# Attention values with the exponentials stationary on the whole array, in a fused attention and expert kernel

## The reference

```python
batch, n_heads, seq, head_dim = (4, 8, 768, 64)
ub = np.sum(np.maximum(q[..., None, :] * k_min, q[..., None, :] * k_max), axis=-1)
top_chunks = np.argsort(np.where(causal, ub, -1e9), axis=-1)[..., -6:]
scores = np.where(sel & causal_by_key, (q @ k.T) / 8, -1e9)
attn = np.exp(scores - max); attn /= attn.sum(-1) + 1e-9
x = (attn @ v)                       # 3072 rows of 512
expert = argmax(x @ w_gate); gate = softmax(x @ w_gate)[expert]
# each expert keeps its 80 rows of highest gate:
out[tok] = gate * (relu(x[tok] @ w1[e]) @ w2[e])
```

## Time and profile before

| | |
|---|---|
| median of 3 runs | 266.83 us (266.33 to 269.99) |
| the profiled execution | 266.53 us |
| its span, first to last instruction | 264.8 us |
| granted clock of the span | 1.000 |

### The profile page before, as it was taken

One profiled execution on the slowest core, in us unless ns is written; L12 is line 12 of the kernel. 1 busy time (PEld: TensorE's weight loads), 2 busy tenths in 40 slices (PEclk: granted clock), 3 DMA queues, 4 the chain that ended last, 5 costly groups with the idle time before them and its releaser, 6 DMA issues.

```text
span 264.8 us, 9133 instructions
## 1 busy us (share of the span) xinstructions
PE 256.2 (97%) x3824; PEld 164.4 (62%) x3824; DVE 213.2 (81%) x582; ACT 149.6 (56%) x227; POOL 211.3 (80%) x280
## 2 busy tenths in 40 slices
PE   7799999999999999999999999999999999989993
PEld 7366566666666566666665666656665657676763
DVE  6886696778989988867889889899999998983332
ACT  2295656565667564647584546564856665873320
POOL 6068889998999899897989898979899971726872
PEclk9999999999999999999999999999999999999999
DMA  9989989999799989997999999999799996941782
GB/s 147 189 145 149 235 225 261 228 187 224 125 208 180 209 145 195 173 219 125 215 160 215 171 190 164 215 162 324 142 207 184 328 212 142 165 103 40 136 167 91
DMA packets 148616, 48.34 MB, mean 183 GB/s; under 512 B 131583, under 2 KB 138870, under 8 KB 148512
## 3 DMA queue, kind: packets, MB, share of 16 engines
q1 hardware_dynamic: 135504, 28.73, 54.1%
q0 software_dynamic: 9936, 18.64, 38.6%
q10 hardware_dynamic: 3136, 0.39, 1.0%
HBM read 57.03 MB, written 11.01 MB: 257 GB/s over the span
## 4 chain that ended last, share of the span: by engine, by line
PE 91%; DVE 3%; ACT 2%; DMA 1%; issue 1%; ACTq 1%; POOL 0%; DVEq 0%
PE OB L637 28%; PE SC L546 27%; PE SC L567 7%; PE OB L1395 4%; PE MM L673 4%; PE SC L1369 4%; PE MM L650 3%; PE OB L721 2%; PE MM L474 2%; PE SC L474 2%; PE MM L513 2%; DMA qn<-in_q_dram 1%; ACT EXB L576 1%; PE MM L712 1%; PE MM L982 1%
## 5 line engine op out<-in xcount | busy, mean ns | idle before, releaser
L576 ACT ACTIVATE EXB<-SC 128x1024 f32<-128x1024 f32 (+1 forms) x87 | 83.1, 966 | 35.6 <-PE SC L546 23.9
L602 POOL TENSOR_TENSOR ES<-ES,EXB 128x512 f32<-128x512 f32 (+1 forms) x81 | 84.4, 1044 | 5.1
L546 PE MATMUL SC<-qT,kT 64*128 64x512 f32 (+3 forms) x476 | 86.3, 464 | 0.1
L637 PE MATMUL OB<-EXB,vn 128*64 128x256 f32 (+3 forms) x704 | 72.9, 361 | 0.0
L637 PEld LDWEIGHTS OB<-EXB,vn 128*64 128x64 f32 x704 | 46.1, 137 | 24.0 <-issue 10.4
L546 PEld LDWEIGHTS SC<-qT,kT 64*128 64x128 f32 x476 | 39.2, 187 | 15.8 <-issue 11.5
L602 POOL TENSOR_TENSOR ES<-EXB 128x512 f32<-128x512 f32 (+1 forms) x29 | 45.3, 1561 | 2.4
L586 POOL TENSOR_SCALAR_AFFINE_SELECT EXB<-EXB 128x256 f32<-128x256 f32 x79 | 34.9, 452 | 5.0 <-ACT EXB L576 5.0
L645 ACT ACTIVATE oT<-OB 128x512 f32<-128x512 f32 (+1 forms) x32 | 15.7, 490 | 40.1 <-PE OB L637 40.1
L567 PE MATMUL SC<-unsT,ind 64*128 64x256 bf16 (+5 forms) x238 | 35.6, 295 | 0.1
L567 PEld LDWEIGHTS SC<-unsT,ind 64*128 64x128 bf16 x238 | 11.8, 95 | 15.9 <-issue 7.1
(11 more groups left out here) (270 smaller groups left out, 405.0 us busy)
## 6 DMA issues: line engine op xcount, KB each, us to landing
w1s<-in_moe_w_dram POOLq DMA_DIRECT2D x8, 1024.0 KB, 8.6
w2s<-in_moe_w_dram POOLq DMA_DIRECT2D x7, 1024.0 KB, 13.9
vn<-in_v_dram SPq DMA_DIRECT2D x32, 192.0 KB, 4.5
kn<-in_k_dram SPq DMA_DIRECT2D x62, 96.0 KB, 3.2
qn<-in_q_dram SPq DMA_DIRECT2D x62, 96.0 KB, 3.5
out_dram<-w1s SPq DMA_DIRECT2D x2, 1536.0 KB, 7.2
out_dram<-out_dram SPq DMA_DIRECT2D x2, 1536.0 KB, 9.8
x_rows<-xp SPq DMA_DIRECT2D x7, 384.0 KB, 3.9
```

The source lines that it names most:

```text
L546: op("pe", lambda: pe.matmul(o, kT[j][pr, ts(kt)], qT[j][pr, q0:q1], start=not flags and (not cols or cols[0] == 0), stop=bool(flags)), r= ...
L576: op("act", lambda: ac.activation(Ex(st, None, 0, W), src, ACTF.Exp, scale=SCALE), r=pk, w=[f"E{st}"])
L602: op(e, lambda: sy.queue[e].tensor_tensor(o, in0, in1, ALU.add), r=[f"E{s2}", f"E{first[0]}"] if first else [f"E{s2}"] + kt, w=kt)
L637: op("pe", lambda: pe.matmul(OB[pr, q0:q1], vn[s][:, kt, h, :], ex, start=(n == 0), stop=last), r=[f"vn{s}{h}", "ES0" if st is None else f ...
```

## The change

Values of pairs 0 to 14 are turned round: each 128x128 block of exponentials is stationary on the whole array, and V with a column of ones (128x65) moves. 21 causal blocks of two heads make 42 products for a pair. The output has queries on partitions, and its 65th column is the key sum. DVE divides by it (`rows_out`), transposes the rows in 32x32 blocks into RT for the logit products, and POOL casts them into xp, which now holds four pairs and is written once for a batch. The logit products (`logits`) are eight products on 64x32 tiles with gate weights that are spread out by four more small DMAs at the start; ACT takes them out, POOL adds them up over a batch, and `logits_sum` folds them once for a batch. All folds of exponentials, the key sum products, the row transposes and the copy of OB to oT go, for pairs 0 to 14. The last pair keeps its way. The ranking sort at `i = 12` is issued behind `rows_out`, one 1 MB expert load (`w2_6`) moves from the end of `i = 14` into `i = 15`, the rows of the last batch stay in xp instead of being read back, and gate work that wrote the PSUM tile MM now writes OB. The core of the diff:

```diff
+                vn = [al(pers, "vn", [128, NT, 2, D + 1]) for _ in range(NB)]
...
+                xp = al(pers, "xp", [128, NT, NPB, 128], BF16)
...
+                WB = bass.AP(oT, 0, [[S, 128], [128, NPB], [32, 4], [1, 32]])
+                SEL = bass.AP(oT, 4 * NPB * 32, [[S, 128], [32, 2], [1, 32]])
+                lgp = bass.AP(oT, 4 * NPB * 32 + 64, [[S, 128], [E * 3, NT], [3, E], [1, 3]])
+                LGT = bass.AP(ES, S, [[2 * S, 128], [192, 2], [1, 192]])
+                LGA = bass.AP(w2s[E - 2], 3 * S, [[FB * Dm, 128], [384, 2], [1, 384]]).bitcast(F32)
...
+                for c in range(4):
+                    src = bass.AP(moe_w_gate.tensor, moe_w_gate.offset, [[E, 32], [128 * E, NPB], [32 * E, 4], [1, E]])
+                    dst = WB[c * 32:c * 32 + 32, :, :, c % 2 * E:c % 2 * E + E]
+                    op("sp", lambda: sp.dma_start(dst, src), r=["Wz"], w=[f"Wb{c}"], dsem=f"d_wb{c}")
...
+                    op("dve", lambda: ve.memset(vn[s][:, :, :, D:D + 1], 1.0), w=[f"von{s}"])
...
-                        for h in range(2):
-                            op("pe", lambda: pe.transpose(MB[h * 64:h * 64 + 64, ts(t)], uns[:, t, h, :], ident_bf[:]),
-                               r=["uns", "ident_bf"], w=["MB"], inc=(t == NT - 2 and h == 1))
+                        op("pe", lambda: pe.transpose(MB[:, ts(t)], uns[:, t, :, :].rearrange("p a b -> p (a b)"), ident_bf[:]),
+                           r=["uns", "ident_bf"], w=["MB"], inc=(t == NT - 2))
...
+                def short(i):
                     return 0 < i < NP - 1
-
-                def short(i):
-                    return mid(i) and i != 12 and (i < NPB or i % NPB < 2)
...
-                            if st == 0 and short(i):
-                                rows(i - 1)
...
                         if i == 0 and st == 2:
-                            short_warm()
+                            keep_warm(2, M0, "M0")
...
-                        if i == NP - 2 and st == (4 if short(i) else 5):
-                            wload(E - 2, 1)
-                        if i < NP - 1:
-                            fold(9 - st if st > 3 and short(i) else st, i=i)
-
-                def values(i, bks=(0, 1), ns=(0, 9), out=True):
+                def values(i):
                     s = i % NB
-                    lists = [AVS_LAST[0] if i == NP - 1 else AVS[0], AVS[1]]
-                    order = AV_ORDER if short(i) else [(bk, n) for bk in bks for n in range(len(lists[bk])) if ns[0] <= n < ns[1]]
-                    for g, (bk, n) in enumerate(order):
+                    blocks = [(st, kt, q, c + q * 128 - q0) for st in ((0, 1, 2, 3, 5, 4) if short(i) else range(6))
+                              for kt, q0, q1, c in STEPS[st] for q in range(q0 // 128, q1 // 128)]
+                    for n, (st, kt, q, c) in enumerate(blocks):
+                        first = all(x[2] // 3 != q // 3 for x in blocks[:n])
+                        end = all(x[2] // 3 != q // 3 for x in blocks[n + 1:])
+                        for h in range(2):
+                            o = q // 3 * 512 + (q % 3 * 2 + h) * (D + 1)
+                            op("pe", lambda: pe.matmul(OB[:, o:o + D + 1], Ex(st, h, c, 128), vn[s][:, kt, h, :],
+                                                       start=first and h == 0, stop=end and h == 1),
+                               r=[f"vn{s}{h}", f"von{s}", f"E{st}"], w=[f"O{q // 3}"], inc=end and h == 1)
...
+                def rows_out(i):
+                    b, p = i // NPB, i % NPB
+                    rden, rk = rd(i)
+                    so = bass.AP(OB, D, [[1024, 128], [512, 2], [D + 1, NT]])
+                    xi = bass.AP(OB, 0, [[1024, 128], [512, 2], [D + 1, NT], [1, D]])
+                    rb = bass.AP(rden, 0, [[NT * 2, 128], [NT, 2], [1, NT]])
+                    rx = bass.AP(rden, 0, [[NT * 2, 128], [NT, 2], [1, NT], [0, D]])
+                    op("dve", lambda: ve.tensor_scalar(rb, so, 1e-9, None, ALU.add), r=["O0", "O1"], w=[rk])
+                    op("dve", lambda: ve.reciprocal(rden[:], rden[:]), r=[rk], w=[rk])
+                    op("dve", lambda: ve.tensor_tensor(RN.rearrange("p (a b c) -> p a b c", a=2, b=NT), xi, rx, ALU.mult), r=["O0", "O1", rk], w=["RN"])
+                    op("dve", lambda: ve.transpose(RT, RN), r=["RN"], w=["RT"])
+                    op("gp", lambda: gp.tensor_copy(xp[:, :, p, :], RN.rearrange("p (t c) -> p t c", t=NT)), r=["RN"], w=[f"xp{p}"])
+                    if p == NPB - 1 or i == NP - 2:
+                        n = (p + 1) * 128
+                        xdst = bass.AP(xd.tensor, xd.offset + b * S * Dm, [[Dm, 128], [128 * Dm, NT], [1, n]])
+                        xsrc = bass.AP(xp, 0, [[NT * Dm, 128], [Dm, NT], [1, n]])
+                        op("sp", lambda: sp.dma_start(xdst, xsrc), r=[f"xp{j}" for j in range(p + 1)], w=[f"xd{b * NPB + j}" for j in range(p + 1)],
+                           dsem="d_xd0")
+                def logits(i):
+                    p = i % NPB
+                    for j in range(4):
+                        for u in range(2):
+                            o = (M0, MBf)[u][j * 32:j * 32 + 32, 0:192]
+                            x = bass.AP(ES, u * 64 * 2 * S + S + j * 32, [[2 * S, 64], [128, NT], [1, 32]])
+                            op("pe", lambda: pe.matmul(o, WB[u * 64:u * 64 + 64, p, j, :], x, start=True, stop=True),
+                               r=["RT", "Wz"] + WBK, w=[("M0", "MB")[u]], inc=(j == 3 and u == 1))
+                def logits_take(i):
+                    src = bass.AP(MM, 0, [[1024, 128], [512, 2], [1, 192]])
+                    if i % NPB == 0:
+                        op("act", lambda: ac.activation(LGA, src, ACTF.Copy), r=["M0", "MB"], w=["LGA"])
+                        return
+                    op("act", lambda: ac.activation(LGT, src, ACTF.Copy), r=["M0", "MB"], w=["RT"])
+                    op("gp", lambda: gp.tensor_tensor(LGA, LGA, LGT, ALU.add), r=["RT", "LGA"], w=["LGA"])
+                def logits_sum(i):
+                    for c in range(4):
+                        op("pe", lambda: pe.matmul(OB[c * 32:c * 32 + 32, 0:192] if i < NP - 1 else M0[c * 32:c * 32 + 32, 0:192], SEL[:, c % 2, :], LGA[:, c // 2, :], start=True, stop=True),
+                           r=["LGA", "Sel0", "Sel1"], w=[lgk(i)], inc=(c == 3))
+                    x = OB if i < NP - 1 else M0
+                    op("dve", lambda: ve.transpose(x[:, 192:384], x[:, 0:192]), r=[lgk(i)], w=["lgT"])
+                def lgk(i):
+                    return "O0" if i < NP - 1 else "M0"
+                def lgv(i):
+                    return (OB if i < NP - 1 else M0)[:, 192:384].rearrange("p (t e) -> p t e", t=NT)[:, :, 0:E]
...
                     scores(i, 0, 2 if i else 3)
+                    if i and i < NP - 1:
+                        rows_out(i - 1)
+                    if i == 12:
+                        sort_rank()
                     if i == NP - 1:
                         sort_rows(True)
...
-                    if i:
-                        sums(i - 1)
-                        scale_lg(i - 1)
-                        if short(i):
-                            scale_rows(i - 1)
+                    turn = live and kk == 0 or i == NP - 1
+                    if turn:
+                        logits(i - 1)
+                        logits_take(i - 1)
...
-                        fold(1, "dve")
-                        fold(2, "dve")
...
+                    if i == NP - 1:
+                        vw_mm()
+                        clear_xg("k", 0)
+                    if turn:
+                        logits_sum(i)
+                        if i < NP - 1:
+                            gate_in(bb)
+                        else:
+                            op("dve", lambda: ve.tensor_copy(lgp[:, :, :, 2], lgv(i)), r=["M0", "lgT"], w=["lgs"])
+                            wload(E - 2, 1)
...
-                        if i == NP - 1:
-                            sort_rank(0)
-                        if mid(i) and not short(i):
-                            rows(i - 1)
-                            if i == 11:
-                                merge(bb, lambda: scale_rows(i - 1))
-                            else:
-                                scale_rows(i - 1)
...
                     scores(i, 4, 6)
-                    if i == 0:
-                        fold(5)
                     if i + 1 < NP:
                         bounds(i + 1)
+                        if i and not turn:
+                            logits(i - 1)
+                            logits_take(i - 1)
...
-                    own_fold(i)
...
                     if i == NP - 2:
                         table(bb)
                         merge(bb)
+                        rows_out(i)
...
                 b = B - 1
                 sums_last()
-                wload(E - 1, 0, ["M0"])
-                early_rows()
+                wload(E - 1, 0, ["S15"])
```

(43 more changed lines are left out.)

209 lines of the change are left out of this document (74 added, 135 removed), and 3 rows, old and new, of the table ADDS.

## The result

The changed kernel takes 331.43 us (median of 4 runs, 330.92 to 331.92) beside 268.41 us for the kernel before on the same chip: 1.238 times as long, 95% interval 1.226 to 1.250; this ratio leaves out the one run of the kernel before, 272.67 us, that fell in a slower state. The forecast was 323 us, 309 to 339. The profiled execution took 330.97 us, its span 329.1 us.

A forecast was written before the change was run, and what follows sets the result against it. PE was taken to bound pairs 0 to 14. Values +71.0, removed PE work -25.8, logits +7.9, turn waits +1.2 and the moved load +2 gave +56.3 on 266.5, so 323 us, range 309 to 339.

The forecast's parts named there:

- The values: Values products of pairs 0 to 14: 84 load-set steps of 111 ns, 9.32 us a pair instead of 4.59, +71.0 us.
- The faster rival: Values: full-array float32 load takes 140 ns like the transposes', step 63 ns, total given as 260 us; chance 0.07.
- Its deciding point: Values of a pair may take 5.57 us, 66 ns a step; below that the kernel is faster than before.
- The slower rival: Values: load and columns do not overlap on the whole array, 169 ns a step, 396 us; chance 0.04.
- The step that failed: PE's time in pairs 0 to 14: gains and losses count in full; scores, masks, bounds net 0.0 us.
- The turns: Pairs 4, 8, 12, 15: logits between score steps cost 1.0 us each; waits for `rows_out` 0.3 each, +1.2 us.
- Head and tail: Outside the pairs: moved load `w2_6` +2 us, six transposes after the loop gone -0.7, together +1.3 us.

The follow-up runs named there:

- The kernel with one half: Changed kernel, but only the first 64 of each block's 128 queries are loaded and multiplied, so output is incomplete: 274.36 us, 1.017 times the kernel before.
- The two halves: Changed kernel, but each 128x128 block of exponentials is loaded as two 64-column blocks into the array's two column halves: 283.25 us, 1.061 times the kernel before.
- the filler: Changed kernel plus products nobody reads, 32 trace rows behind the second score step in each of 11 pairs: 339.41 us, 1.251 times the kernel before.

## Why the prediction was right, and where it was off

**The values** were right by their mechanism and to 1%: load 192 ns (forecast 188), step 112 (111), +71.9 us (+71.0). That the step is the load's is shown: it doesn't move when columns of V go, and it falls to 60, about half, when half of the load's columns go. The step taken from the score products on 64 rows of the array held for 128.

**The faster rival** fell with the load: the 140 ns of the transposes are not those of a product. Its deciding point, 5.57 us of values, was too generous. By the measured terms all but the values come to -7.6 us, 0.51 a pair, so the values could take 4.64 + 0.51 = 5.15 us. The kernel with one half is near that point, with 5.17 us of values on average; it is still 1.7% slower than before, and the waits told above account for more than the 4 us that this is. The two halves have 6.09 with their holes.

**The slower rival** is out by the step: 112 ns, not 169, and the same with 33, 49 and 65 columns, so the columns lie beside the load. The rule named with it, the Trainium skill, "TensorE: Matmul & The Clock Gate", "Part 3: Packing small matmuls — row/col tiling", by which a load overlaps products in flight only when its row group differs, doesn't hold for these float32 products either: every load takes the same rows, all of the array, and one of 192 ns starts every 112.

**The step that failed** is the sentence that what PE gains or loses is gained or lost in full, with the scores, masks and bounds priced at nothing net. They cost 4.0 us more: 2.9 in the eleven pairs in which the filler stands, 0.7 in the three at a turn, 0.4 in pair 0. In those eleven the scores and masks alone are 4.4 us longer and the bounds 1.5 shorter. The filler shows the cause for most of the 4.4: it takes 3.2 back. Between the second and third step PE had the sums to do while ACT made its exponentials, and without them it waits there. The rest is read from the trace and wasn't tried, such as 0.2 us in each of the pairs 5, 9 and 13, in which the scores wait for ACT's copy of the gates (L813, 1.7 us of load waits with the filler and without it).

**The turns** were sized well: logits with their sum took 0.93 to 1.09 us (forecast 1.0), and scores, masks and bounds grew by 0.3, 0.3 and 0.1 us in pairs 4, 8 and 12 (0.3 each). In the other pairs a run of logits took 0.46 us and not 0.35, 1.2 us in all eleven; the bounds ahead of it got 0.14 shorter, 1.5 us in all, which the forecast did not have. That these two nearly cancel is luck. **Head and tail** cost 3.2 us instead of 1.3, with the 2.1 us wait for the first gather and, behind it, a stretch at a mean clock of 0.79, where 1.00 was forecast. That the moved load causes that wait was the theory; as moving `w1_7` only shifted it, which transfer is to blame stays open. POOL came to 32%, not 40%, with no effect.

## What to carry to other kernels

Price a matmul by the longer of its load and its columns, and take the load from rows of the same type and the same number of weight columns: turning the operands round made 84 loads of 128 columns out of 48 of 64 in a pair, and that outweighed all the work saved. Before counting a removed run of products as a gain, look at which engine's result the next run needs: a run between two steps that wait for another engine is partly free. And when a step is cut into more, shorter instructions, look at the holes that end shortly after an instruction packet.

## What the runs showed of the hardware

- **The clock can fall while PE is never idle.** With 33 or 49 moving columns under the same 112 ns loads, the granted clock went from 1.00 to 0.50 in every run of values, while PE was busy throughout, and steps of 112 ns became 213; with 65 columns and the same step it stayed at 1.00 through all 15 runs of values. Moving less made the kernel over 90 us slower. Why the clock falls is not shown.
- **Two column halves load and multiply side by side:** 168 steps of 64-column loads take the 5.05 us that 84 take alone.
- **Holes follow instruction packets when steps are short:** with steps of 30 ns, each a load and a product, nine holes of 0.5 to 1.9 us end 2.2 to 2.5 us after a packet of the instruction queue starts; with steps of 60 ns none came, and slower products among the short ones left five. That PE runs out of instructions there is read from this and from the 66.8 us with twice as many; it is not shown.
- **A wait need not show as idle time:** PE counts as busy for 17.42 of 17.52 us in a pair, yet 0.23 us of waits for ACT lie in it. The starts of the rows show them; the waits of the weight loads overstate them, 15.8 us less with the filler where 3.2 came back.
